# Six two-way levels in place of three four-way levels for the decayed attention scores, and all keys of the first two units raised on GpSimd

## The reference

```python
# decayed linear attention, per batch b (4) and head h (8), 768 tokens, 48 features
state = alpha[t, :, None] * state + outer(k[t], v[t]);   y[t] = q[t] @ state
# then, on the 3072 tokens of 384 features:
h = relu(x @ w1[e]);  x2 = sum_e p[e] * (h @ w2[e])      # 4 experts, 1024 wide
h = x2 @ w_in;  out = (h - tanh(h)) @ w_out              # 2048 wide
```

## Time and profile before

| what | us |
|---|---|
| median of 3 runs | 1383.19 (1381.79 to 1383.29) |
| the profiled execution, its own time | 1381.91 |
| its span (first to last instruction) | 1380.1 |
| TensorE busy, matmuls (10177 records) | 1338.2 (97%) |
| VectorE busy (1767) | 874.3 (63%) |
| ScalarE busy (1072) | 573.4 (42%) |
| GpSimd busy (274) | 277.2 (20%) |
| chain that ended last | TensorE 89%, VectorE 7%, ScalarE 2% |

### The profile page before, as it was taken

One profiled execution on the slowest core, in us unless ns is written; L12 is line 12 of the kernel. 1 busy time (PEld: TensorE's weight loads), 2 busy tenths in 40 slices (PEclk: granted clock), 3 DMA queues, 4 the chain that ended last, 5 costly groups with the idle time before them and its releaser, 6 DMA issues.

```text
span 1380.1 us, 25841 instructions
## 1 busy us (share of the span) xinstructions
PE 1338.2 (97%) x10177; PEld 1121.9 (81%) x10177; DVE 874.3 (63%) x1767; ACT 573.4 (42%) x1072; POOL 277.2 (20%) x274
## 2 busy tenths in 40 slices
PE   3699999999999999999999999999999999999999
PEld 3578788988878888878898887888887889888888
DVE  8984855994654875465687565497556378323285
ACT  1525346843214751414662323374231476211175
POOL 4666654004022001313001403100221000000000
PEclk8799999999999999999999999999999999999999
DMA  7389797856655656565655655664665465655552
GB/s 217 92 306 321 240 323 242 322 212 219 211 196 197 231 181 218 181 211 196 242 183 179 222 194 199 207 229 169 216 211 172 161 220 189 222 185 200 180 193 89
DMA packets 104680, 289.08 MB, mean 209 GB/s; under 512 B 9936, under 2 KB 64432, under 8 KB 104560
## 3 DMA queue, kind: packets, MB, share of 16 engines
q1 hardware_dynamic: 104416, 287.23, 60.9%
q10 hardware_dynamic: 144, 0.20, 0.1%
HBM read 242.52 MB, written 42.52 MB: 207 GB/s over the span
## 4 chain that ended last, share of the span: by engine, by line
PE 89%; DVE 7%; ACT 2%; issue 1%; DMA 0%; DVEq 0%
PE bank L662 14%; PE bank L663 13%; PE bank L664 13%; PE bank L687 9%; PE bank L688 9%; PE bank L689 9%; PE bank L713 4%; PE bank L711 4%; PE bank L712 4%; PE bank L575 4%; PE bank L616 2%; PE bank L553 1%; DVE RG L1166 1%; PE bank L588 1%; DVE GG L1136 1%
## 5 line engine op out<-in xcount | busy, mean ns | idle before, releaser
L887 ACT ACTIVATE HH<-GG 128x512 fp32r<-128x512 f32 x192 | 121.2, 631 | 631.4 <-PE bank L689 509.2
L662 PE MATMUL bank<-XB,RG 128*128 128x512 f32 x864 | 348.5, 403 | 4.7 <-DVE GG L1109 2.2
L663 PE MATMUL bank<-XB,RG 128*128 128x512 f32 x864 | 339.4, 393 | 0.0
L664 PE MATMUL bank<-XB,RG 128*128 128x512 f32 x864 | 338.3, 392 | 0.0
L1109 DVE SCALAR_TENSOR_TENSOR GG<-bank,PB 128x512 f32<-128x512 f32 x192 | 133.4, 695 | 310.3 <-PE bank L664 310.0
L687 PE MATMUL bank<-HH,RG 128*128 128x512 f32 x576 | 224.3, 389 | 0.0
L688 PE MATMUL bank<-HH,RG 128*128 128x512 f32 x576 | 224.2, 389 | 0.0
L689 PE MATMUL bank<-HL,RG 128*128 128x512 f32 x576 | 224.0, 389 | 0.0
L1320 POOL TENSOR_TENSOR KU<-KU,TOT 128x256 f32<-128x256 f32 x88 | 68.5, 805 | 699.3 <-PE bank L575 699.3
L662 PEld LDWEIGHTS bank<-XB,RG 128*128 128x128 f32 x864 | 162.1, 188 | 45.9 <-issue 4.2
L664 PEld LDWEIGHTS bank<-XB,RG 128*128 128x128 f32 x864 | 162.2, 188 | 35.4
(11 more groups left out here) (129 smaller groups left out, 1676.8 us busy)
## 6 DMA issues: line engine op xcount, KB each, us to landing
RG<-scratch SPq DMA_DIRECT2D x240, 768.0 KB, 4.3
scratch<-RG SPq DMA_DIRECT2D x48, 768.0 KB, 5.3
VS<-vp SPq DMA_DIRECT2D x11, 768.0 KB, 6.0
WS<-w SPq DMA_DIRECT2D x32, 192.0 KB, 3.4
PB<-probs SPq DMA_DIRECT2D x6, 1024.0 KB, 7.0
AU<-qka SPq DMA_DIRECT2D x11, 512.0 KB, 5.3
R<-qka SPq DMA_DIRECT2D x11, 512.0 KB, 5.2
KU<-qka SPq DMA_DIRECT2D x11, 512.0 KB, 6.2
```

The lines of the kernel that those rows point to most:

```text
L662: nc.tensor.matmul(out, w1(g, 0, kt), x_part(m, 0, kt), start=(kt == order[0]), stop=False)
L663: nc.tensor.matmul(out, w1(g, 0, kt), x_part(m, 1, kt), start=False, stop=False)
L664: last = nc.tensor.matmul(out, w1(g, 1, kt), x_part(m, 0, kt), start=False, stop=(kt == order[-1]))
L887: nc.scalar.activation(HH[:, h_slot(g)], GG[:, h_slot(g)], ACT.Copy).then_inc(high, 1)
```

## The change

The levels become six, with h = 1, 2, 4, 8, 16, 32, and each joins sub-blocks two by two. A level raises the keys of the first of two sub-blocks by the total decay of the second, and the queries of the second by the total of the first: one operation of 512 columns each, in place. The queries no longer have distant copies: one tensor QS of 1024 columns replaces R0 and R2, and units of the main sequence alternate between two of them. The matmuls of a level take the second sub-blocks alone as moving columns: 32 matmuls of 32 columns, in one step, with the same 64x64 weights and the same order over the quarters as diagonal. The six levels stand at steps 1, 2, 4, 5, 7, 8; GpSimd raises the keys and VectorE the queries in the same step. pick is two operations of 256 columns to a level. The table of decays takes six operations in place of nine. In the prologue GpSimd raises all keys of both units, and VectorE none; ScalarE's order becomes lay(0), lay(1), swap_totals(1), probabilities, join(0), carry_own(0), carry_last(1), join(1), and TensorE does the turns of both units before deltas(0). rotate(AHEAD, 0) ahead of slot 0 goes.

```diff
-LEVELS = [1, 4, 16]
+LEVELS = [1, 2, 4, 8, 16, 32]
+SCORES_AT = [1, 2, 4, 5, 7, 8]
-SW = CH // 4 * (ROWS - 1)
+SW = CH // 2
@@ tensor
+            def scores(u, level):
+                if level == 0:
+                    pe.wait_ge(spread[own(u)], turn_of(u) + 1)
+                else:
+                    pe.wait_ge(keys_up[own(u)], NL * turn_of(u) + level)
+                    pe.wait_ge(rotated[own(u)], NL * turn_of(u) + level)
+                bank_free(u, 2 + 2 * level)
+                bank_free(u, 3 + 2 * level)
+                _, second = halves(queries(u)[:, :], LEVELS[level])
+                n = SW // LEVELS[level]
+                for m in range(2 * UC):
+                    for k in range(2):
+                        c = (m // UC * 2 + k) * UC + m % UC
+                        for o, keys, q in crossed(u, c, k):
+                            last = nc.tensor.matmul(fill_bank(u, 2 + 2 * level + k)[o, m * SW:m * SW + SW], keys,
+                                                    second[q, c * n:c * n + n, :], start=True, stop=True)
+                        if m == 2 * UC - 1:
+                            last.then_inc(filled[own(u)], 1)
...
             diagonal(0)
-            scores(0, 0, 0)
+            scores(0, 0)
             diagonal(1)
...
+            scores(1, 0)
+            for level in range(1, NL):
+                for u in range(AHEAD):
+                    scores(u, level)
             turn(0, 0)
             turn(0, 1)
-            scores(1, 2, 0)
-            scores(1, 2, 1)
-            deltas(0)
             turn(1, 0)
             turn(1, 1)
+            deltas(0)
@@ scalar
-            join(0)
             lay(1, 0)
...
+            join(0)
             carry_own(0)
@@ vector
+            def rotate(u, level):
+                first, _, _ = tables(u, level)
+                dve.wait_ge(filled[own(u)], filled_at(u, 3 + 2 * level))
+                if level:
+                    dve.wait_ge(tabled[own(u)], NL * turn_of(u) + level)
+                _, q = halves(queries(u)[:, :], LEVELS[level])
+                nc.vector.tensor_tensor(q, q, first.to_broadcast([P, SPAN[level] // 2, LEVELS[level]]),
+                                        ALU.mult).then_inc(rotated[own(u)], 1)
...
+            pick(0, 0)
+            for level in range(1, NL):
+                rotate(0, level)
+                tabulate(1, level, level + 1)
+                pick(1, level - 1)
+                rotate(1, level)
+                pick(0, level)
+            pick(1, NL - 1)
             probabilities()
...
-            rotate(AHEAD, 0)
@@ gpsimd
+            def raise_keys(u, level):
+                _, second, _ = tables(u, level)
+                pool.wait_ge(filled[own(u)], filled_at(u, 3 + 2 * level))
+                if level:
+                    pool.wait_ge(tabled[own(u)], NL * turn_of(u) + level)
+                k, _ = halves(KU[own(u)][:, :], LEVELS[level])
+                nc.gpsimd.tensor_tensor(k, k, second.to_broadcast([P, SPAN[level] // 2, LEVELS[level]]),
+                                      ALU.mult).then_inc(keys_up[own(u)], 1)
...
             def attention(u, step):
-                if step in (3, 6, 9):
-                    raise_keys(u, step // 3 - 1)
+                if step in SCORES_AT:
+                    raise_keys(u, SCORES_AT.index(step))
...
-            spread_queries(1)
-            raise_keys(0, 0)
-            spread_distant(1)
-            tabulate(1, 1, 9)
-            raise_keys(0, 1)
-            raise_keys(0, 2)
-            raise_keys(1, 1)
-            raise_keys(1, 2)
+            for level in range(NL):
+                raise_keys(0, level)
+                raise_keys(1, level)
```

More of the change, by code:

```diff
@@ L62, with mask_at @@
 REST = C0 - C1 * C1 / (4 * C2)
[L65 to L66 removed]
+def mask_at(level):
+    return level * SW
 def level_masks():
@@ L266, in program, with halves, queries @@
         block = ctx.enter_context(nc.Block())
[L268 to L276, removed]
-        def tables(u, level):
[L279 to L283, removed]
+        def halves(ap, h):
+            pairs = ap.rearrange("p (n two h) -> p n two h", two=2, h=h)
+            return pairs[:, :, 0, :], pairs[:, :, 1, :]
+        def queries(u):
+            return QS[2 if own(u) else turn_of(u) % 2]
+        def tables(u, level):
+            t = total(u, level).rearrange("p (n two) -> p n two", two=2)
+            return t[:, :, 0:1], t[:, :, 1:2], total(u, level + 1).rearrange("p (n a) -> p n a", a=1)
         def total(u, level):
@@ L289, in total @@
                 return T64[u % 2][:, :]
[L290 to L302, removed]
+            at = sum(SPAN[1:level])
+            return TOT[own(u)][:, at:at + SPAN[level]]
         def fill_bank(u, k):
@@ L556, in diagonal @@
                             last.then_inc(filled[own(u)], 1)
[L558 to L572, removed]
-                        c = (2 * half + n) * UC + m
-                        for o, keys, q in crossed(u, c, n):
-                            last = nc.tensor.matmul(fill_bank(u, k + n)[o, m * SW:m * SW + SW], keys,
-                                                    rows[q, c * groups:c * groups + groups, h:ROWS * h],
-                                                    start=True, stop=True)
-                        if m == UC - 1:
+            def scores(u, level):
[15 more added lines that the diff above has]
+                        if m == 2 * UC - 1:
                             last.then_inc(filled[own(u)], 1)
@@ L1274, in _, with tabulate @@
         def _(pool):
-            def tabulate(u, first=0, last=9):
-                n = 9 * turn_of(u)
-                for i in range(first, last):
-                    t, two, three = tables(u, i // 3)
-                    if i:
-                        pool.wait_ge(tabled[own(u)], n + i)
-                    if i % 3 == 0:
-                        out, a, b = two, t[:, :, 0:3], t[:, :, 1:4]
-                    elif i % 3 == 1:
-                        out, a, b = three, two[:, :, 0:2], t[:, :, 2:4]
-                    else:
-                        out, a, b = total(u, i // 3 + 1).rearrange("p (n a) -> p n a", a=1), three[:, :, 0:1], t[:, :, 3:4]
-                    nc.gpsimd.tensor_tensor(out, a, b, ALU.mult).then_inc(tabled[own(u)], 1)
+            def tabulate(u, first=0, last=NL):
+                n = NL * turn_of(u)
+                for level in range(first, last):
+                    one, two, both = tables(u, level)
+                    if level:
+                        pool.wait_ge(tabled[own(u)], n + level)
+                    nc.gpsimd.tensor_tensor(both, one, two, ALU.mult).then_inc(tabled[own(u)], 1)
             def spread_queries(u):
```

246 lines of the change are left out of this document (63 added, 183 removed).

## The result

The changed kernel takes 1393.81 us, the median of four runs (1391.34 to 1395.93); the kernel before took 1382.49 beside it. The ratio is 1.0084 (95% interval 1.0059 to 1.0109), so it is slower by 11.3 us, more than the 0.2% that can be told from no change. The profiled execution took 1391.34 us with a span of 1389.6, 9.5 us over the span before.

A forecast was written before the change was run, and what follows sets the result against it. TensorE, busy 1295.5 of 1300 us from 80 us on, bounds the kernel; in the prologue the chain between engines. +16.2 - 4.0 + 1.4 = +13.6 on 1381.91 gives 1395.5, plus 1.28 for the median: 1396.8 us, range 1378 to 1406.

The forecast's parts named there:

- Score block: Steady part, TensorE: weight loads make a new score block cost the diagonal's price, +0.27 us each, +16.2 us over 60.
- columns decide: Rival, score blocks: two loads into a quarter overlap, a block takes 0.12 us less; 1374 us, faster; chance 0.14.
- in between: Rival, score blocks: records start at the pace of the deltas, +0.05 us a block; 1384 us, no measurable difference; chance 0.12.
- VectorE and GpSimd hidden: Steady part: both engines' changed work costs nothing, hidden under TensorE's slots of about 4.1 us.
- late keys in every unit: Rival: VectorE holds up GpSimd's raise, level 1 scores wait in step 2, 1 us a unit; 1407 us; chance 0.07.
- Prologue: Before slot 0: five levels of 4.5 us each let lay(0) begin near 39.7 instead of 43.68, giving 4.0 us.
- The lock: Prologue: VectorE's two-SBUF-input operations wait out GpSimd's, so raises, rotates and table run in turn, 3.9 us a level.
- First slots: Slots 0 to 2: two TensorE waits replaced by one of about 4.5 us for GpSimd's keys, costing 1.4 us more.

The follow-up runs named there:

- cols16: Changed kernel, score matmuls from unit 2 on streaming 16 moving columns in place of 32, weights as they are: 1393.12 us (one run).
- cols64: Changed kernel, score matmuls from unit 2 on streaming 64 moving columns in place of 32: 1394.70 us (one run).
- trim: Changed kernel, score matmuls of level h loading only the first 64 - h weight columns (not at level 0 of units 0 and 1): 1383.53 us, ratio 1.0014.
- keys_first: Changed kernel with GpSimd's low parts of weights 6 and 7 behind slot 1's raise in place of ahead of it: 1389.08 us, ratio 1.0048.
- rotate_later: Kernel before the change, with VectorE's rotate(2, 0) behind the scale of slot 2, not ahead of slot 0: 1383.83 us, ratio 1.0014.
- load32_all: Changed kernel, score matmuls loading 32 weight columns in place of 64, in the prologue too from level 1 on: 1366.8 us.
- load32: Changed kernel, score matmuls from unit 2 on loading 32 weight columns in place of 64, prologue left at 64: 1372.83 us (one run).

## Why the prediction was right, and where its sizes were off

**Score block: right.** The forecast was a block at the diagonal's price, since weight loads decide; starts of 15 ns, loads of 134 ns and 1.7 us between the neighbours were named beforehand, and 14.6, 134 and 1.72 came. The rival "columns decide" falls with cols16 and cols64, "in between" with them. Only the size was off: +1.33 us a unit, 13.3 over ten units, in place of 16.2. The new block costs 0.03 us less than the diagonal's (I had allowed 0.01), and the old one 1.48 rather than 1.47 us at most places, so it is +0.24 between MoE matmuls of 512 columns. Of unit 3's six blocks two stand behind the second network's matmuls of 384 columns instead, and there it is +0.21: 4 x 0.24 + 2 x 0.21 = 1.38, close to the 1.33. Two of the rivals' sums were off. By the forecast's own figures 64 new records cost what 32 old ones do at 31 x 20.9 / 63 = 10.3 ns a record, not 12.8, and at the pace of the deltas a block costs 63 x 11.7 - 31 x 20.9 ns = +0.09 us, not +0.05, so that case stood at 1386 rather than 1384. Neither enters the forecast.

**VectorE and GpSimd hidden: right.** From slot 4 on TensorE waits once for VectorE (0.70 us at 288 us, where the kernel before waits 0.64) and never for GpSimd; the rival of late keys in every unit has no row. What I missed is a wait of the kernel before for VectorE's picks, in unit 3, which is gone: -0.9. That fewer picks are the reason is likely, but no run tests it.

**Prologue: right in mechanism but for one term, -5.1 for -4.0.** lay(0) came at 39.22 for the 39.7 forecast, a level took 4.33 us for 4.5, and ScalarE's chain from there to high_x is as long as before (16.74 us). The other 0.7 lie behind it, between high_x and slot 0. The lock is there as forecast, and an allowance on its 3.9 us was needed. But what fills part of it is a term that the sum did not have: TensorE's stops for its instructions, which 64 records a block bring once a level. In the changed kernel they were short; in trim, whose prologue differs by shorter loads alone, they were longer, and lay(0) came 1.2 us later. That 4.5 came so near 4.33 is in part luck. One row was misread without effect: the 0.22 us of the earlier trace rows are for a pick of 192 columns, not 128; a pick of 256 took 0.38 to 0.65 us where 0.36 was assumed.

**First slots: right in mechanism, +2.2 for +1.4.** The wait for the scale went, and one for GpSimd's keys came. scores(2, 1) started 12.2 us after slot 0's start for the 12.7 forecast; the forecast's own terms add up to 12.5. That is closer than its terms: ScalarE's split of weight 7 began 7.2 us after slot 0 and not 8.5, while GpSimd's split (2.06 us for 1.85) and raise (1.95 for 1.3, a rotate beside it) took longer. The wait itself was 2.9 us and not 4.5, because TensorE ran slot 0 at the low clock and came to it late; but the same clock fell again behind the wait, some 1.5 us. I had priced waits by their length and not by the slow matmuls behind them. The 2.2 are what is left of the -1.6 at unit 2's deltas when the prologue's -5.1 and one unit's 1.33 are taken off. keys_first shows that the order on GpSimd causes the wait; rotate_later shows that the rotate moved to slot 2 wins nothing, since the waits move with it.

**Sum.** 13.3 - 0.9 - 5.1 + 2.2 = +9.5 us in the span, where the forecast had +13.6. The median lies 2.5 us above the profiled execution and not 1.3. Together: 1393.8 for 1396.8. The first slots' 2.2 are a remainder, so that the sum closes is no proof of its terms; the errors were -2.9 (blocks), -0.9, -1.1, +0.8 and +1.2, and those of opposite sign helped.

## What to carry to other kernels

Count the weight loads of small matmuls as well as their columns: with the fp32 matmuls of this case four 64x64 quarters in turn start a record every max(load of the tile, time of its moving columns) / 4, with 0 to 2 ns over, and fewer moving columns in more matmuls pay only while the columns are the longer of the two. Where loads decide, drop the weight columns that no wanted output needs. And where an engine's wait ahead of TensorE is replaced by another, price what TensorE's clock does behind it too, and look which of two operations, VectorE's or GpSimd's, starts first. And where a long stretch holds nothing but small matmuls, look for idle time of TensorE in the middle of a block: there its own instructions can come too late.

## What the runs showed of the hardware that was not expected

- Starts every 8.6 ns: 64 records of 32 moving and 32 weight columns over four quarters took 0.76 us. The Trainium skill's floor of about 25 ns between starts, which the prediction weighed, does not hold there by a factor of three.
- Behind waits of 2.7 and 2.9 us TensorE ran eight to nine matmuls at 1.2 GHz and not 2.4 (granted 0.52 and 0.50), and behind 2.39 us as well; behind 1.33 us (keys_first) and behind 3.1 us (trim, load32_all) at the second block it did not, while in load32 it did behind 3.1 us at the same block. Which wait is followed by a slow stretch these runs do not settle.
- In the prologue TensorE stops up to 2.1 us in the middle of a block of small matmuls and goes on 1.2 to 1.5 us after a 16 KB packet of the instruction queue q8 has ended, in every trace that has such idle time; a record costs that queue 128 bytes.
- Prologues of the same instructions differ by some 2 us from one execution to another: slot 0 begins at 61.85 in the changed kernel, at 61.72 in keys_first and at 63.93 in load32. Terms of the prologue taken from one profile hold no closer than that.
